# First maxima stored ahead of the third head's deal, and the first transposed scores ahead of the next pair's scores

## The reference

```python
scores = scale * np.matmul(q, k.transpose(0, 1, 3, 2))
thresh = np.max(scores, axis=-1, keepdims=True) - tau
scores = np.where(scores >= thresh, scores, -1000000000.0)
attn = softmax(scores)                # written out in the reference
x = attn @ v                          # heads side by side: 2304 x 512
x = ((x @ w_a) * (x @ w_b)) @ w_out   # 512 -> 1536 -> 512
h = x @ w_in                          # 512 -> 1024
out = (layernorm(h * softmax(h)) * g_ln) @ w_out2
```

## Time and profile before

| | |
|---|---|
| device time, 3 runs | median 999.86 us (999.68 to 1000.23) |
| the profiled execution's own time | 1000.2 us |
| its span, first to last instruction | 998.4 us |
| PE busy | 976.0 us, 98% of the span |
| DVE, ACT, POOL busy | 529.9, 415.6, 253.9 us |
| all that PE waited in the first 75 us | 11.3 us, of which 6.7 ahead of its first matmul |

### The profile page before, as it was taken

The page is one execution under the profiler, slowest core; times in us unless marked ns, Lnnn a source line. Parts: engine busy times, 40 slices in busy tenths (PEclk is TensorE's granted clock), DMA queues, the critical chain, the costliest instruction groups (busy, mean ns, idle before and its releaser), DMA issues.

```text
span 998.4 us, 16512 instructions
## 1 busy us (share of the span) xinstructions
PE 976.0 (98%) x5844; PEld 925.7 (93%) x5844; DVE 529.9 (53%) x863; ACT 415.6 (42%) x739; POOL 253.9 (25%) x242
## 2 busy tenths in 40 slices
PE   5999999999999999999999999999999999999997
PEld 5999999999998999999999999999999778888886
DVE  6788788878778644322222222222223766556664
ACT  3777777777778543212112112112122422223221
POOL 2777787777878100000000000000000000000000
PEclk9999999999999999999999999999999999999999
DMA  6666666666761543110010010000021100000000
GB/s 176 160 159 162 156 160 160 158 158 157 173 143 53 168 130 96 32 33 1 0 32 0 0 32 0 0 0 0 0 84 43 41 22 21 21 24 28 21 22 32
DMA packets 51566, 71.31 MB, mean 71 GB/s; under 512 B 14552, under 2 KB 24920, under 8 KB 51536
## 3 DMA queue, kind: packets, MB, share of 16 engines
q1 hardware_dynamic: 51536, 70.94, 27.6%
HBM read 33.25 MB, written 5.32 MB: 39 GB/s over the span
## 4 chain that ended last, share of the span: by engine, by line
PE 92%; issue 3%; DVE 2%; DMA 1%; SPq 1%; ACT 1%; POOL 0%; POOLq 0%
PE PS L1114 12%; PE PS L1131 10%; PE PS L1132 10%; PE PS L1133 10%; PE PS L1076 9%; PE PS L1078 8%; PE PS L1199 5%; PE PS L1198 5%; PE PS L1200 5%; PE PS L1257 3%; PE PS L1259 3%; PE PS L1258 3%; PE PS L1233 3%; PE PS L1231 3%; PE PS L1232 3%
## 5 line engine op out<-in xcount | busy, mean ns | idle before, releaser
L532 POOL TENSOR_TENSOR p_lo<-prob,p_hi 128x576 fp32r<-128x576 f32 x144 | 207.9, 1445 | 50.8 <-ACT p_hi L612 48.9
L1076 PE MATMUL PS<-ops 128*128 128x288 f32 x642 | 182.2, 305 | 14.8 <-DVE ops L911 6.7
L1131 PE MATMUL PS<-x_hi,w_ab_rolled 128*128 128x384 f32 x576 | 192.5, 334 | 0.2 <-DVE w_ab_rolled L867 0.2
L1133 PE MATMUL PS<-x_hi,w_ab_rolled 128*128 128x384 f32 x576 | 192.4, 334 | 0.0
L1132 PE MATMUL PS<-x_lo,w_ab_rolled 128*128 128x384 f32 x576 | 192.4, 334 | 0.0
L1078 PE MATMUL PS<-ops 128*128 128x288 f32 x642 | 177.6, 298 | 0.0
L950 DVE TENSOR_TENSOR gate<-gate,PS 128x384 f32<-128x384 f32 x72 | 39.9, 554 | 251.9 <-ACT gate L716 251.9
L716 ACT ACTIVATE gate<-PS 128x384 f32<-128x384 f32 x72 | 35.4, 492 | 266.7 <-PE PS L1133 266.7
L1076 PEld LDWEIGHTS PS<-ops 128*128 128x128 f32 x642 | 122.6, 191 | 23.9 <-issue 12.3
L835 DVE TENSOR_REDUCE neg_max<-PS 128x1 f32<-128x576 f32 x144 | 108.5, 755 | 59.9 <-PE PS L1078 59.7
L1078 PEld LDWEIGHTS PS<-ops 128*128 128x128 f32 x642 | 122.8, 191 | 0.0
(11 more groups left out here) (91 smaller groups left out, 1523.6 us busy)
## 6 DMA issues: line engine op xcount, KB each, us to landing
qk_raw<-qkT_dram SPq DMA_DIRECT2D x32, 288.0 KB, 3.1
ops<-qk_hi SPq DMA_DIRECT2D x62, 144.0 KB
ops<-qk_hi SPq DMA_DIRECT2D x31, 288.0 KB
ops<-qk_lo SPq DMA_DIRECT2D x62, 144.0 KB
v_raw<-v_tiles_dram SPq DMA_DIRECT2D x32, 160.0 KB, 2.6
xT<-head_sb SPq DMA_DIRECT2D x32, 144.0 KB, 3.3
out_dram<-o_sb SPq DMA_DIRECT2D x18, 256.0 KB, 2.0
stage<-inverse_dram SPq DMA_DIRECT2D x20, 192.0 KB, 3.9
```

Of the source, the lines that this page charges most:

```text
L532: pool.tensor_tensor(p_lo[:, s, :], prob[:, s, :], p_hi[:, r, :].bitcast(F32), ALU.subtract).then_inc(p_lo_done, 1)
L1076: pe.matmul(ps[:, b, 0:HALF], weights[0][:, r, own], moving[0][:, r, cols], start=(n == 0), stop=False)
L1131: pe.matmul(bank, w[:, 0, :], x_hi[:, k, :], start=(k == 0), stop=False)
L1133: ins = pe.matmul(bank, w[:, 1, :], x_hi[:, k, :], start=False, stop=(k == NK - 1))
```

## The change

On SP's queue, at the start, `store_max(0, 0)` moves ahead of `deal_high(0, 2, ...)`, and `deal_low(0, 2)` moves behind `load_max(0, 0)`. On PE, in the very first slot of the first step, `scores_t` of head 0 comes ahead of `scores` of head 2, with an explicit wait for all nine reductions of the first pair in front (it writes a PSUM tile that the last of them read). Nothing is added or removed; all other slots stay as they were.

```diff
             deal_low(0, 1)
             load_qk(0, 3)
             load_v(0, 0)
+            store_max(0, 0)
             deal_high(0, 2, qk_hi_done)
-            store_max(0, 0)
-            deal_low(0, 2)
 
             sp.wait_ge(s_done, NT)
             load_max(0, 0)
+            deal_low(0, 2)
             load_v(0, 1)
...
                     ei, ee, es = early_tile(i, e, s)
-                    if exists(ei, ee):
+                    if isinstance(i, int) and 2 * i + e + s == 0:
+
+                        pe.wait_ge(max_done, SLOTS)
+                        scores_t(i, e, s)
                         scores(ei, ee, es)
-                    scores_t(i, e, s)
+                    else:
+                        if exists(ei, ee):
+                            scores(ei, ee, es)
+                        scores_t(i, e, s)
```

## The result

The changed kernel takes 1002.27 us (median of 16 runs, 1000.97 to 1002.46), the kernel before 1000.24 us in 16 runs beside it (999.68 to 1002.34). The ratio is 1.0017, 95% interval 1.001 to 1.0023: some 2 us slower, where +0.4 was forecast, and outside the stated range. The profiled execution took 1002.35 us. One of the 11 executions of the kernel with only the queue changed, further down, took 1070.18 us at a granted clock of 0.85; its ratio leaves that one out.

A forecast was written before the change was run, and what follows sets the result against it. PE was taken to bound the kernel, working unbroken from 28.35 us. Only head 2's late low parts cost: +1.12 us, +0.41 after the cushion; 1000.2 + 0.4 = 1000.6, less 0.34 for the median: 1000.3 us, range 999.4 to 1001.3.

The forecast's parts named there:

- the sum: Costs of the start-up changes added to the profiled execution: 1000.2 + 0.4 = 1000.6 us, forecast 1000.3 us for the median.
- fourth rival: PE's pauses at 19.0 and 20.9 us drop its clock until 30 us: +4 us, 1004 us; chance 0.03.
- the cushion: PE's 0.71 us wait for head 3's low parts at slot 4 (28.35 us); PE may come that much later at no cost.
- The swap costs nothing: PE, slot 0 of the first step: next scores 0.64 us later, covered by 0.71 us of waiting at slot 4; cost 0.
- The load of the maxima lands by 19.8: SP's queue: load issued at about 17.5 us, landing 2.3 us later, ahead of the 20.07 needed; cost 0.
- Head 2's low parts land at 21.1: Second low DMA issued at about 18.4 us, taking 2.7 us; head 2's scores start at 21.24 for 20.12, +1.12 us.
- The term +0.41: Slot 4 on PE: 28.76 us against 28.35, what head 2's late low parts cost after the 0.71 us wait is used up.
- The estimate of 2.3 us by the fit: Head 2's low DMA: 2.0 us fixed plus bytes over 436 GB/s, 2.3 us for 144 KB; landing at 20.7, no cost.
- Head 3's operands stay hidden: They start some 0.25 us later and would release PE at 28.6 us, just hidden behind PE's own +0.41.
- the store of head 1's maxima has slack: SP's queue: 1.31 us of slack for the store issued at 23.14, against a delay of 1.12; cost 0, but close.
- A gain from head 1's low parts: PE's 0.16 us wait at 13.29 us might shrink with less queued data: up to -0.16 us, counted as nothing.
- all lateness behind it reaches the end: From slot 4 at 28.35 us PE works without a break; what it is later by, the end is later by.

The follow-up runs named there:

- swap-only profile: Profile of the kernel before with only PE's order changed (`scores_t` of head 0 ahead of `scores` of head 2), SP's queue as before; 1000.82 us against 1000.40, ratio 1.0003.
- fillers: The changed kernel plus 16 matmuls computing nothing needed in PE's pauses around slot 0 (8, 2 and 6); 1001.26 us against 1000.40 for the kernel before, ratio 1.0012.
- warm kernel before: The kernel before plus matmuls computing nothing needed: 20 at PE's start, 4 in each of three early pauses, 8 and 2 around slot 0; 1000.01 us, ratio 0.9999.
- both kernels with both moves: The changed kernel, 1002.27 us, and the changed kernel plus early matmuls computing nothing needed, with 8, 2 and 6 around slot 0, 999.47 us.

## Why the prediction was wrong

The step that failed is the clock: the sum has no term for it. It stands only as the fourth rival, with a chance of 0.03, and in the changed profile it cost 1.61 us, more than all that the sum did count. The rival's mechanism and its sign were in the text, and two of the three pauses. Its price was too high (+4 us): it took some 45 matmuls at the lower level where 24 ran so, and took only the cushion off, where another 1 us went into waits that were there anyway. It was kept small by the sentence that PE had paused 1.14 us ahead of 20.12 and did not fall. That row was true and too little: the changed kernel pauses three times in 4 us (1.35, 0.34 and 0.85 us), and falls. The third pause, up to 23.11 us, is the one that the prediction did not see. "TensorE: Matmul & The Clock Gate" of the Trainium skill, Part 1, says that idleness throttles the clock; this case's trace now agrees, granted 0.54 and 0.50 after these pauses.

Point by point:

- *The swap costs nothing.* Wrong. It was costed by the start of each product alone (+0.64 us at the next scores, inside the cushion). That it takes away PE's work beside the reduction of slot 0 was not seen. In the swap-only profile the pause that this makes (0.85 us for 0.32), behind one of 1.21 us, is followed by the clock's fall. That kernel's time, +0.4 us, is not clear of nothing; its slot 4 is 0.80 us late.
- *The load of the maxima lands by 19.8.* Wrong by half a microsecond: it released PE at 20.39, which with 0.14 us for PE's start is a landing at 20.25, 2.8 us after its issue, and not 2.3. It cost nothing by itself, since PE still had to wait 0.34 us for head 2's low parts behind it. In the swap-only profile too it, and not DVE, released slot 0 (20.38): the load went out at 18.74 us there, behind the store.
- *Head 2's low parts land at 21.1.* They landed at 21.36 by the chain: issued 0.36 us later than worked out, and landed in 2.60 us against 2.7. The term +0.41 is 1.34 - 0.71 = +0.63 in the changed profile and, with the clock held by fillers, +0.9 at slot 4 and +0.86 us in the time. The estimate of 2.3 us by the fit in the Trainium skill, page "DMA: Bandwidth & Descriptors", section "Anatomy of one DMA", is short of the measured 2.60 by 0.3 us; the page gives that fit for DMAs that GpSimd issues, and these are SyncE's.
- *Head 3's operands stay hidden; the store of head 1's maxima has slack.* Right in the changed kernel: 23.20 for 23.14, and slot 4 without a wait.
- *A gain from head 1's low parts.* None: PE was released at 13.33, before at 13.29.
- *The cushion of 0.71 us, and that all lateness behind it reaches the end.* Right: span less slot 4 is 970.0 us in both.

So the loss is 0.6 to 0.9 us of late operands and reductions less the cushion, and 1.2 to 1.6 us of clock: the changed profile splits its 2.24 us as 0.63 and 1.61, the fillers' runs split +2.03 us as 0.86 and 1.17, across two sessions. Late operands alone would have left the time inside the stated range (1000.24 + 0.86 = 1001.1 us). In single executions of the changed kernel whose mean granted clock was 1.00, two of 16, the times were 1000.97 and 1001.81 us; the others show 0.995 to 0.998 and lie mostly at 1002.1 to 1002.5, with three at 1001.1 to 1001.7.

Open: why the queue alone costs 1.3 us in the plain kernel (its one profile was not a typical start), what adds 0.5 us behind slot 4 in two of the kernels with extra matmuls, and why the mean granted clock is below 0.999 in 9 of 30 executions of the kernel before and not in its profile.

## What to carry to other kernels

Where an engine's clock depends on its activity, cost a reordering by the pauses that it makes as well as by the waits: list the pauses in the stretch before and after, and ask what the engine did beside each wait that now does nothing. A product that seems free to move may be the cover of a reduction. And before judging a reordering of a start-up as bad, hold the clock with extra matmuls: here the same change went from +2.0 us to a difference, -0.5 us by the medians, that these runs cannot tell from nothing.

## What the runs showed of the hardware

- In the changed profile the clock fell with no pause over 1.35 us between matmuls, after three close together (granted 1.00, then 0.54 and 0.50), and in the swap-only profile after two, of 1.21 and 0.85 us (granted 0.66). In the profile of the kernel before it stayed at 1.00 through pauses of 1.14 and 0.32 us. In the changed profile PE then worked nearly without a break from 23.11, and the clock was back at about 29.4 us.
- At the start the matmuls run 0.24 us apart while the granted clock reads 1.00; the column shows only a fall after the first rise. The spacing of equal matmuls is the safer reading.
- Sixteen matmuls added to PE's pauses brought the changed kernel from +2.03 us to +0.86 us over the kernel before (each in its own session), and slot 4 from 30.59 to 29.25 us.
- A 16 KB store issued behind 576 KB took 2.5 us (plain kernel before) to 5.4 us (warm kernel before) until its load went out. Issued ahead of them, with the load right behind them, it was at most 2.7 us in both kernels with both moves.
